# A recurrence and two dense stages: the low part of x of the first three tiles from TensorE and ScalarE, and another order of the work

## The reference

```python
# 1: a recurrence over the positions t, per batch and head
cur = np.einsum('bhd,bhe->bhde', u[None] * kt, vt)
y[:, :, t] = np.einsum('bhd,bhde->bhe', rt, state + cur)
state = wt[:, :, :, None] * state + np.einsum('bhd,bhe->bhde', kt, vt)
# 2: x = y, heads side by side; w_in is 384 x 1024, w_out 1024 x 384
h = np.maximum(x @ w_in, 0.0)
conv_out = sum over k of conv_w[k] * (h shifted by k - 1 positions)
x = (h * sigmoid(conv_out)) @ w_out
# 3: w_ch1 is 384 x 1536, w_ch2 1536 x 384
xn = (x - mu) / np.sqrt(var + 1e-06) * g_ln
out = x + np.maximum(xn @ w_ch1, 0.0) @ w_ch2
```

## Time and profile before

| what | value |
|---|---|
| median of 3 runs | 345.31 us (344.94 to 346.1) |
| the profiled execution | 345.43 us |
| its span, first to last instruction | 343.7 us |
| TensorE busy over the span | 331.2 us (96%) |
| VectorE busy | 244.1 us (71%) |
| ScalarE busy | 141.5 us (41%) |
| GpSimd busy | 69.3 us (20%) |
| granted TensorE clock | 1.00 throughout |

### The profile page before, as it was taken

The page is one execution under the profiler, slowest core; times in us unless marked ns, Lnnn a source line. Parts: engine busy times, 40 slices in busy tenths (PEclk is TensorE's granted clock), DMA queues, the critical chain, the costliest instruction groups (busy, mean ns, idle before and its releaser), DMA issues.

```text
span 343.7 us, 8546 instructions
## 1 busy us (share of the span) xinstructions
PE 331.2 (96%) x3184; PEld 310.8 (90%) x3184; DVE 244.1 (71%) x525; ACT 141.5 (41%) x339; POOL 69.3 (20%) x160
## 2 busy tenths in 40 slices
PE   6987999999999999999999999999999999999996
PEld 6866868999998999999899999899999999998996
DVE  3997789899897777597768598787785612766222
ACT  2215765535474222374212274412374412754110
POOL 4654001242402032000322110322130100100100
PEclk9999999999999999999999999999999999999999
DMA  9958625913144320344521353140000100000101
GB/s 151 220 130 250 220 72 178 255 22 57 19 74 68 52 69 6 47 62 51 115 49 19 45 84 45 48 91 2 2 4 0 41 7 2 0 2 1 49 0 46
DMA packets 89251, 22.79 MB, mean 66 GB/s; under 512 B 83423, under 2 KB 87674, under 8 KB 89210
## 3 DMA queue, kind: packets, MB, share of 16 engines
q1 hardware_dynamic: 87984, 21.84, 31.7%
q10 hardware_dynamic: 1226, 0.41, 0.6%
HBM read 19.87 MB, written 2.36 MB: 65 GB/s over the span
## 4 chain that ended last, share of the span: by engine, by line
PE 79%; DVE 2%; ACT 1%; issue 0%; DVEq 0%; ACTq 0%
PE hid L620 12%; PE hid L621 11%; PE hid L624 11%; PE acc L632 7%; PE acc L633 7%; PE acc L640 3%; PE acc L639 3%; PE pair_a L1388 2%; PE pair_a L632 2%; PE pair_a L633 2%; PE pair_b L633 2%; PE pair_b L632 2%; PE pair_b L640 2%; PE pair_a L639 2%; PE y_ps L1425 2%; PE y_ps L1431 1%
## 5 line engine op out<-in xcount | busy, mean ns | idle before, releaser
L1060 ACT ACTIVATE g_hi<-hid 128x256 fp32r<-128x256 f32 x58 | 22.2, 383 | 93.8 <-PE acc L640 80.8
L620 PE MATMUL hid<-xc_hi,w_hi 128*128 128x256 f32 x216 | 54.9, 286 | 1.0 <-DVE xc_lo L1287 0.5
L1307 DVE SCALAR_TENSOR_TENSOR g_lo<-hid,g_hi 128x256 fp32r<-128x256 f32 x58 | 24.4, 420 | 42.9 <-ACT g_hi L1060 42.9
L1081 DVE SCALAR_TENSOR_TENSOR cg<-h_all,cols,cg 128x256 f32<-128x256 f32 x96 | 46.2, 483 | 9.8 <-ACT cg L1023 8.9
L621 PE MATMUL hid<-xc_hi,w_lo 128*128 128x256 f32 x216 | 53.0, 277 | 0.0
L620 PEld LDWEIGHTS hid<-xc_hi,w_hi 128*128 128x128 f32 x216 | 40.6, 188 | 3.5 <-issue 1.6
L621 PEld LDWEIGHTS hid<-xc_hi,w_lo 128*128 128x128 f32 x216 | 40.6, 188 | 0.0
L632 PE MATMUL acc<-w_hi,g_hi 128*128 128x384 f32 x116 | 40.0, 345 | 0.0
L620 PE MATMUL hid<-x_hi,win_hi 128*128 128x258 f32 (+1 forms) x144 | 38.4, 295 | 1.2 <-POOL x_hi L888 1.2
L633 PE MATMUL acc<-w_lo,g_hi 128*128 128x384 f32 x116 | 39.1, 337 | 0.0
L621 PE MATMUL hid<-x_hi,win_lo 128*128 128x258 f32 (+1 forms) x144 | 36.7, 283 | 0.0
(11 more groups left out here) (196 smaller groups left out, 760.6 us busy)
## 6 DMA issues: line engine op xcount, KB each, us to landing
v_in<-in_v SPq DMA_DIRECT2D x12, 192.0 KB, 3.3
lent<-in_moe_w_ch SPq DMA_DIRECT2D x6, 384.0 KB, 4.5
lent<-in_moe_w_in SPq DMA_DIRECT2D x6, 256.0 KB, 4.5
lent<-in_moe_w_out SPq DMA_DIRECT2D x4, 384.0 KB, 7.2
w_two<-in_w SPq DMA_DIRECT2D x6, 192.0 KB, 6.0
k_two<-in_k SPq DMA_DIRECT2D x6, 192.0 KB, 4.6
bv<-in_k SPq DMA_DIRECT2D x6, 192.0 KB, 3.5
ruk<-in_r SPq DMA_DIRECT2D x6, 192.0 KB, 3.4
```

Source lines behind the costliest of these rows:

```text
L620: pe.matmul(out_ps, wh, xh, start=i == 0, stop=False)
L1060: act.activation(relu_parts(n, j)[0], hid[j % 2][:, 0:GP], ACT.Relu)\
L1081: dve.scalar_tensor_tensor(out=cv, in0=h[:, t:t + GP], scalar=cols[:, t * JF + j:t * JF + j + 1], in1=cv, op0=ALU.mult, op1=ALU.add).then_ ...
L1307: dve.scalar_tensor_tensor(out=low, in0=hid[j % 2][:, 0:GP], scalar=0.0, in1=high.bitcast(F32), op0=ALU.max, op1=ALU.subtract).then_inc(s_ ...
```

## The change

The low part of x of tiles 0, 1 and 2 (`LOW_BY_TENSOR = 3`) is no longer subtracted by VectorE. A new item `xl` does it: TensorE multiplies minus the identity by `x_hi` and adds that to what stands in the bank `y_ps`, so that the bank holds y - x_hi, and ScalarE copies it to `x_lo`. `minus` is made once at the start by ScalarE. Tiles 3 to 11 are worked as before.

```diff
+        LOW_BY_TENSOR = 3
+        minus = sb("minus", [P, P], F32R)
...
+            act.wait_ge(s_eye, 2)
+            act.activation(minus[:, :], ident[:, :], ACT.Copy, scale=-1.0).then_inc(s_minus, 1)
...
+                elif kind == "xl":
+                    act.wait_ge(m_rest, n + 1)
+                    act.activation(x_lo[s][:, :, 1 + b * P:1 + (b + 1) * P],
+                                   y_ps[:, 0:DM].rearrange("p (a s) -> p a s", s=P), ACT.Copy)\
+                       .then_inc(s_xlo, 1)
...
-                elif kind == "x":
+                elif kind == "x" and n >= LOW_BY_TENSOR:
                     dve.wait_ge(s_xhi, n + 1)
...
+                elif kind == "xl":
+
+                    pe.wait_ge(s_minus, 1)
+                    pe.wait_ge(s_xhi, n + 1)
+                    pe.matmul(y_ps[:, 0:DM].rearrange("p (a s) -> p a s", s=P), minus[:, :],
+                              x_hi[s][:, :, 1 + b * P:1 + (b + 1) * P], start=False, stop=True,
+                              skip_group_check=True).then_inc(m_rest, 1)
```

`FIRST` is written anew. Its second half, from the scores of tile 1 on, before and after:

```diff
-                 ("mask", 1), ("sc", 1), ("r", 2), ("scan2", 2), ("ruk", 2), ("x", 0), ("bv", 2), ("ke", 1),
-                 ("load_k", 3), ("cols", 0), ("load_v", 3), ("mid", 2), ("k", 2), ("state", 1), ("fetch", 5),
-                 ("sums", 2), ("weights", 0), ("x", 1), ("mask", 2), ("weights", 1), ("middle", 2),
-                 ("weights", 2), ("weights", 3), ("load_r", 3), ("fetch", 16), ("weights", 4), ("kv", 1),
-                 ("fetch", 17), ("x", 2), ("fetch", 18), ("y", 1), ("weights", 5), ("fetch", 19), ("fetch", 6),
-                 ("fetch", 7), ("sc", 2), ("y", 2)]
+                 ("mask", 1), ("sc", 1), ("scan2", 2), ("ruk", 2), ("x", 0), ("weights", 0), ("xl", 0),
+                 ("bv", 2), ("ke", 1), ("load_k", 3), ("cols", 0), ("load_v", 3), ("mid", 2), ("fetch", 5),
+                 ("k", 2), ("state", 1), ("r", 2), ("sums", 2), ("x", 1), ("y", 1), ("mask", 2), ("middle", 2),
+                 ("weights", 1), ("kv", 1), ("weights", 2), ("weights", 3), ("load_r", 3), ("fetch", 16),
+                 ("weights", 4), ("fetch", 17), ("fetch", 18), ("fetch", 19), ("xl", 1), ("weights", 5),
+                 ("fetch", 6), ("fetch", 7), ("sc", 2), ("x", 2), ("y", 2), ("xl", 2)]
```

More of the change, by code:

```diff
@@ new lines, in rwkv_mlp_kernel @@
+        FIRST = [("load_w", 0), ("ru", 0), ("load_k", 0), ("scan1", 0), ("load_v", 0), ("scan2", 0), ("w", 0),
+                 ("r", 0), ("load_w", 1), ("load_w", 2), ("load_k", 1), ("fetch", 0), ("fetch", 1),
+                 ("load_r", 1), ("load_r", 2), ("fetch", 2), ("mid", 0), ("load_w", 3), ("ruk", 0),
+                 ("scan1", 1), ("k", 0), ("load_v", 1), ("bv", 0), ("scan2", 1), ("w", 1), ("ru", 1),
+                 ("ke", 0), ("sums", 0), ("ruk", 1), ("sc", 0), ("w", 2), ("middle", 0), ("middle", 1),
+                 ("mask", 0), ("mid", 1), ("kv", 0), ("sums", 1), ("fetch", 3), ("fetch", 4), ("load_k", 2),
+                 ("k", 1), ("ru", 2), ("bv", 1), ("r", 1), ("y", 0), ("load_v", 2), ("scan1", 2), ("state", 0),
+                 ("mask", 1), ("sc", 1), ("scan2", 2), ("ruk", 2), ("x", 0), ("weights", 0), ("xl", 0),
[4 more added lines that the diff above has]
+                 ("fetch", 6), ("fetch", 7), ("sc", 2), ("x", 2), ("y", 2), ("xl", 2)]
@@ L369, in rwkv_mlp_kernel @@
         AFTER = {
             ("conv", 0, 1): [("load_w", 4)],
[L371 to L376, removed]
+            ("hidden", 0, 2): [("fetch", 8)],
+            ("hidden", 0, 3): [("load_k", 4), ("fetch", 9)],
@@ L377, in rwkv_mlp_kernel @@
+            ("hidden", 0, 4): [("fetch", 10)],
+            ("project", 0, 1): [("load_v", 4), ("middle", 3)],
+            ("project", 0, 2): [("fetch", 11), ("ru", 3), ("weights", 6), ("weights", 7)],
+            ("conv", 0, 6): [("fetch", 12)],
             ("conv", 0, 7): [("weights", 8)],
-            ("project", 0, 6): [("weights", 9), ("w", 3)],
+            ("project", 0, 6): [("weights", 9), ("w", 3), ("fetch", 13)],
             ("norm", 0): [("k", 3), ("ke", 2), ("r", 3)],
             ("turn", 0): [("kv", 2), ("scan1", 3)],
-            ("hidden2", 0, 0): [("state", 2), ("scan2", 3), ("ruk", 3)],
@@ L382, in rwkv_mlp_kernel @@
-            ("hidden2", 0, 1): [("bv", 3), ("mid", 3)],
-            ("project2", 0, 0): [("fetch", 14), ("weights", 10), ("weights", 11), ("w", 4), ("weights", 12)],
+            ("hidden2", 0, 0): [("state", 2), ("ruk", 3), ("scan2", 3)],
+            ("hidden2", 0, 1): [("bv", 3)],
+            ("project2", 0, 0): [("fetch", 14), ("weights", 10), ("mid", 3), ("weights", 11), ("w", 4),
+                                 ("weights", 12)],
             ("project2", 0, 1): [("ke", 3), ("weights", 13)],
@@ L402, in rwkv_mlp_kernel @@
             ("conv", 1, 1): [("load_k", 6), ("ruk", 5), ("sc", 5), ("row_k", 6)],
-            ("hidden", 1, 3): [("kv", 4), ("state", 4), ("pads_k", 6)],
-            ("gate", 1, 3): [("bv", 5)],
-            ("hidden", 1, 6): [("pads_r", 6)],
+            ("conv", 1, 3): [("kv", 4), ("state", 4)],
+            ("conv", 1, 5): [("bv", 5)],
+            ("hidden", 1, 6): [("pads_r", 6), ("pads_k", 6)],
             ("conv", 1, 6): [("load_v", 6), ("load_v", 7)],
@@ L438, in rwkv_mlp_kernel @@
             ("turn", 2): [("kv", 7)],
-            ("result", 1): [("ru", 9)],
             ("hidden2", 2, 1): [("scan2", 8)],
-            ("project2", 2, 0): [("r", 8), ("state", 7)],
-            ("hidden2", 2, 3): [("mid", 8)],
+            ("project2", 2, 0): [("r", 8), ("state", 7), ("ru", 9)],
             ("project2", 2, 1): [("sums", 8)],
             ("hidden2", 2, 4): [("load_v", 8)],
-            ("project2", 2, 2): [("mask", 8), ("middle", 8)],
-            ("add", 1, 0): [("ruk", 9), ("row_k", 9)],
[5 rows of a table removed]
+            ("project2", 2, 2): [("mid", 8), ("middle", 8)],
@@ L452, in rwkv_mlp_kernel @@
+            ("add", 1, 0): [("ruk", 9)],
[5 rows of a table added]
             ("hidden2", 2, 10): [("mid", 9), ("load_v", 9), ("y", 8), ("x", 8)],
             ("project2", 2, 9): [("sc", 9), ("bv", 9), ("mask", 9)],
-            ("conv", 3, 0): [("state", 8), ("load_w", 10)],
-            ("hidden", 3, 1): [("kv", 8)],
+            ("conv", 3, 0): [("state", 8)],
+            ("conv", 3, 1): [("kv", 8)],
+            ("conv", 3, 2): [("load_w", 10)],
             ("project", 3, 0): [("w", 10)],
-            ("conv", 3, 4): [("middle", 9), ("middle", 10)],
@@ L458, in rwkv_mlp_kernel @@
[L458 to L461, removed]
+            ("conv", 3, 4): [("middle", 9)],
+            ("gate", 3, 4): [("load_r", 10), ("middle", 10)],
+            ("hidden", 3, 6): [("row_k", 10)],
+            ("gate", 3, 5): [("ru", 10)],
+            ("conv", 3, 7): [("r", 10), ("y", 9)],
+            ("project", 3, 4): [("row_r", 10), ("x", 9), ("load_k", 10)],
@@ L476, in rwkv_mlp_kernel @@
             ("hidden2", 3, 10): [("mask", 11), ("kv", 10), ("sc", 11)],
             ("hidden2", 3, 11): [("state", 10)],
-            ("hidden", 4, 1): [("late", 3, 8)],
-            ("gate", 4, 0): [("bv", 11)],
+            ("hidden", 4, 1): [("bv", 11), ("late", 3, 8), ("row_r", 11)],
             ("project", 4, 4): [("y", 11)],
```

49 lines of the change are left out of this document (25 added, 24 removed), and 16 rows, old and new, of the table AFTER.

## The result

| what | before | after |
|---|---|---|
| median of 20 runs each | 344.93 us (343.97 to 346.4) | 345.87 us (345.27 to 347.67) |
| ratio after to before | | 1.0029, 95% interval 1.0015 to 1.0042 |
| the profiled execution, its span | 345.43, 343.7 us | 345.79, 344.1 us |
| low passes of ("hidden", 0, 0) start | 31.93 | 32.59 |

What follows compares the result with a forecast made beforehand. TensorE sets the pace once stage 2 runs, so the start's gain goes through: 0.11 (earlier product) plus 0.41 (x_lo not late) is 0.52, the rest 0; 345.43 becomes 344.9, or 344.8 from the median; range 344.0 to 346.2.

Steps and rivals of the forecast that it cites:

- Up to r 2: TensorE's start: xl 0, ke 1, cols and k 2 fill 1.59 of idle time; r 2 still starts at 21.18.
- The new loads of k at the start are of data that is needed later than it comes: Loads at the start: the new loads of k delay nothing; priced at 0 with the later edits, 0.3 either way.
- the moved items pass one neighbour each: Later order, AFTER: the moves change nothing on TensorE's path; priced at 0, with 0.3 either way.
- bv 2 at 0.83 when a mask follows the sum: GpSimd's bonus values of tile 2: 0.83 long instead of 1.21, so y 2 starts at 27.20 instead of 27.27.
- the fifth piece lands after 29.6: Sign that the prediction is wrong: w_in's fifth piece, expected at 29.06, lands later than 29.6.
- The distance from the low passes to the end: From the low passes of the first stage 2 product to the end: 311.8 as before, within 0.3.
- middle 0: ScalarE's copy, now behind ruk 1: 0 to 0.1 late, taken as 0; 0.65 if as long as a whole product.
- the two operations taken out before the sum: VectorE before the sum of tile 2: their gain is eaten by a weight split and a wait; the sum 0.31 later.
- The fifth piece at ScalarE: weights 5 before x 2 waits for its piece of w_in: 0.05 of loss, 1.7 if it takes 5.8 to land.
- GpSimd goes first: Rival, chance 0.08: ruk 2 gets in before VectorE's split of weights 0; a loss of 0.1, 345.4.
- The piece late: Rival, chance 0.13: w_in's fifth piece lands late and holds x 2 on ScalarE; up to 1.2 of loss, 346.5.
- A later wait goes too: Rival, chance 0.12: TensorE's 0.72 wait for VectorE's centring at group 3's turn also goes; gain 1.24, 344.1.

Runs made afterwards that it cites:

- e1: The changed kernel with the load of k of tile 2 issued before fetches 3 and 4: 345.33 us, ratio 0.9993 to before.
- e3: The changed kernel with both edits, the load of k of tile 2 early and mid 3 back: 344.73 us, ratio 0.998 to before.
- e2: The changed kernel with mid 3 back where it was, before weights 10 on VectorE: 345.87 us, ratio 1.0017 to before.
- e7: e3 with weights 5 on ScalarE behind xl 2 instead of before x 2: 344.39 us, ratio 0.9975 to before.
- e4: The changed kernel's order without xl items, VectorE subtracting the low part of x of all tiles: 347.88 us, ratio 1.007 to before.
- e5: The kernel before with the xl items put in, kv 1 and y 1 listed earlier, without the new order: 345.49 us, ratio 1.000.
- e10: e8 with the scores of tile 2 ahead of xl 1 on TensorE: 344.11 us, ratio 0.9954 to before.
- e9: The kernel before with the load of k of tile 2 ahead of fetches 3 and 4 on SyncE: 346.09 us, ratio 1.0009.
- e8: e7 with kv 1 ahead of y 1 on TensorE and xl 1 ahead of weights 1 on ScalarE: 344.54 us, ratio 0.9972 to before.
- e6: The changed kernel with the whole AFTER of before, only FIRST and the xl items new: 345.90 us, ratio 1.0019 to before.

## Why the prediction was wrong

**The step that failed** is the first, "Up to r 2": "xl 0, ke 1, cols and k 2 now stand in the 1.59 of idle time before r 2", "r 2 still waits for mask 1 and starts at 21.18". k 2 was moved past r 2 and costed as work that fills a hole; that it also waits, for its load, was not looked up. The load's two rows were in the trace of before: issued at 17.45, 4.1 to land, 21.55 in all, 0.37 after the time that was given to r 2, and k 2 itself takes 0.5 ahead of r 2. Even by these rows r 2 would have stood near 22.05. The sentence "The new loads of k at the start are of data that is needed later than it comes" speaks of the loads that moved; that of k 2 did not move, its reader did, and no sentence looks at it. The term was 0; it measured 1.16 at r 2 (22.34 against 21.18), and e1 and e3 show that it is this load: with it early the wait is gone and the low passes are 1.01 earlier (e3's against those of the changed kernel). The other links of the sum were nearly right; this term turned 0.52 of gain into 0.66 of loss at the low passes.

**The second** is "the moved items pass one neighbour each", priced at 0 with 0.3 either way. It was reasoned from TensorE's full windows and not from the slack of each item. Mid 3 had 1.8 us of it, and it passes two instructions of VectorE, not one: a low part of stage 3 (0.41), and weights 10, which takes 1.02 and waits 0.47 for ScalarE. It stands 2.0 later than the shift alone would put it (61.79 less 59.09 and 0.66). It cost 0.5 at its place (e2), 0.18 in the medians, which alone is inside the prediction's 0.3.

**What was right.** y 1's length (2.1, said: 2.2), the sum 1.06 behind state 1, bv 2 at 0.83 when a mask follows the sum, the piece landing 4.0 after issue (said: 4.1), x_lo late by only 0.1. The sign "the fifth piece lands after 29.6" came true (30.09), but with the chain 1.03 late and not by a slow landing. The distance from the low passes to the end is 311.5, within 0.3 of the 311.8. middle 0 took 0.29 at 17.65 and delayed nothing. e3, the changed kernel with the two losses mended, has y 2 within 0.02 of the forecast and the low passes 0.17 behind it: ScalarE's copy of x_lo 2 ends at 31.17, not at 31.02, and GpSimd's edge copy behind it at 31.43, not 31.27. One reading was wrong and changed nothing: "the two operations taken out before the sum" are one, since the subtraction of x 1 stood behind the sum (26.36). The fifth piece at ScalarE was the right doubt, and its size depends on the landing: from y 2 to x_hi 2 it is 2.26 in the earlier trace rows and in e7, 2.38 in the changed kernel and 2.43 in e3 (so 0.12 and 0.17 lost; the forecast's own times, 27.20 and 29.58, make 2.38 too, and its "0.05" counts from the 29.53 of before), but in e1's profile, where the piece took 5.0 to land, x_hi 2 came 1.1 later than that.

**The rivals.** "GpSimd goes first" did not happen: the split started at 22.46, ruk 2 at 22.50, and it was ruk 2 that took longer, 1.49 against 1.01. That agrees with the Trainium skill, "SBUF — State Buffer", section "Who interferes with whom": the one that comes first holds the shared ports to its end. ruk 2 ended at 23.99, long before the sum that reads it (26.64), so nothing came of it. In e4's profile the order was the other way: ruk 2 at 22.49 took 0.99, and the split behind it, at 22.89, took 1.14 in place of 0.67. The piece late did not happen (4.0; it was 5.0 in e1's profile). "A later wait goes too" happened in part in this one profile: the wait at the turn of group 3 went from 0.72 to 0.34, on a chain that was 1.16 late. The mechanism named was the right one: GpSimd's product and the centring were parted by some 0.4, and the centring fell from 1.23 to 0.84. But they stand differently from kernel to kernel, with either `AFTER`.

## What to carry to other kernels

When an item is moved forward past a neighbour, look up not only how long it takes but when each thing that it waits for is there, its DMA's issue and landing above all; a transfer that nobody waited for becomes a bound as soon as its reader is early. A hole in an engine's timeline can hold only work whose inputs are ready in it. And moving work to another engine and reordering the queues should be judged together: here each, as it was run, lost (e4, with the late load still in it, and e5, at full clock); together, with the load and mid 3 mended, they stood 0.2 below before, which is not clear of the noise, and with three more links put right 0.75 (e10). How much of that is the early load's own is open (e9).

## What the runs showed of the hardware

**TensorE's clock falls in the start of some executions.** e1's profiled execution has the granted clock at 0.81 and then 0.50 (1.2 of 2.4 GHz) behind a stretch in which TensorE was nearly idle. Its windows:

```profile
29.00:31.00 2.00, 0.26 (x12) 0.00 (x0) 1.13 (x3) 1.01 (x2) 0.01 (x1) 1.00 1.05 352
31.00:32.00 1.00, 0.93 (x5) 0.73 (x6) 0.33 (x1) 0.48 (x1) 0.38 (x1) 1.00 1.06 392
32.00:33.00 1.00, 1.00 (x7) 0.85 (x6) 0.00 (x0) 0.01 (x1) 0.93 (x3) 0.81 1.11 404
33.00:34.00 1.00, 1.00 (x6) 1.00 (x6) 0.00 (x0) 0.66 (x2) 0.46 (x1) 0.50 1.04 387
```

In e9's it fell earlier, behind the hole before r 2:

```profile
19.00:21.00 2.00, 0.66 (x23) 0.41 (x14) 2.00 (x4) 0.22 (x1) 1.60 (x3) 1.00 0.89 279
...
23.00:24.00 1.00, 1.00 (x17) 0.94 (x16) 0.93 (x3) 0.55 (x2) 0.63 (x3) 0.50 0.00 0
```

Products of 128x258 went from 0.28 to 0.42 long in e1, and an execution with one such fall is 1.2 to 1.9 us longer (medians of e5 and e9, the ends). The kernel before has the same hole before r 2 in its profile and kept its clock, so a hole of that length does not always bring a fall. Counted over all executions with a clock on record, beside the longest single wait of TensorE from 17 us to the low passes in the kernel's profile:

| kernels | longest wait | executions with a fall |
|---|---|---|
| e8, e10 | 0.72, 0.85 | 0 of 24 |
| changed, e2, e3, e6, e7 | 1.17 to 1.21 | 16 of 67 |
| before, e5, e9 | 1.59 | 40 of 114 |
| e4 | 1.73 | 5 of 7 |
| e1 | 1.80 (its fifth piece took 5.0) | 3 of 12 |

Shorter holes go with fewer falls in the main, but before (31 of 90), e5 (2 of 12) and e9 (7 of 12) differ with the same longest wait, and each wait is that of one profile. That the holes are the cause is not shown; no run tested it by itself. The falls also move the plain medians: by these e10 is 0.9 below before, and 0.75 at full clock.

**How long an instruction of GpSimd or VectorE lasts depends on what the other does beside it, and so on the order.** bv 2 lasts 0.83 with a mask beside it (the changed kernel, e3, e7, e10) and 1.21 with a split beside it (e5, before); ruk 2 lasts 1.01 or 1.49, and the small edge copies 0.19 or up to 0.70. It holds the other way too: VectorE's split lasts 0.67, or 1.14 behind ruk 2 (e4), and its centring 0.42, or up to 1.23 beside a product of GpSimd. None of these is a change in the instruction.
